# Linear-attention stage on host layouts by token and by dimension: no transposes of k and r, block-diagonal state per head pair, decays on ScalarE

## The reference, cut to what matters

```python
# B=2, H=8, S=768, D=48
for t in range(S):
    kt, vt, rt = k[:, :, t], v[:, :, t], r[:, :, t]
    cur = einsum('bhd,bhe->bhde', u * kt, vt)
    y[:, :, t] = einsum('bhd,bhde->bhe', rt, state + cur)
    state = w * state + einsum('bhd,bhe->bhde', kt, vt)
x = y, as rows of 384 per token          # 1536 tokens
x = moe(x)       # 8 experts of 384x1024 and 1024x384
x = moe2(x)
```

## Time and profile before

| | us |
|---|---|
| median of 3 runs | 395.46 (395.17 to 395.58) |
| the profiled execution's own time | 396.4 |
| its span | 394.3 |
| first score (unit 0) starts at | 15.67 |
| score of unit 2 starts at | 27.98 |
| score of unit 11 starts at | 76.22 |
| one unit from there on, from score to score | 5.36 |
| first expert product starts at | 96.47 |

### The profile page before, as it was taken

The page is one execution under the profiler, slowest core; times in us unless marked ns, Lnnn a source line. Parts: engine busy times, 40 slices in busy tenths (PEclk is TensorE's granted clock), DMA queues, the critical chain, the costliest instruction groups (busy, mean ns, idle before and its releaser), DMA issues.

```text
span 394.3 us, 10784 instructions
## 1 busy us (share of the span) xinstructions
PE 366.7 (93%) x3406; PEld 356.9 (91%) x3407; DVE 209.6 (53%) x539; ACT 133.0 (34%) x230; POOL 184.5 (47%) x303
## 2 busy tenths in 40 slices
PE   4689999988999999999999999879999999999990
PEld 4579999977899999999999999769999999999990
DVE  4356666689688655555555577474214454244210
ACT  2447554410544222222222252105215555255220
POOL 6798999815455532323232334152434524444311
PEclk9999999998999999999999999699999999999996
DMA  6898774146999511111111321139349998492000
GB/s 128 142 353 185 164 161 100 40 129 169 402 405 404 215 40 40 40 40 40 40 40 40 112 114 40 13 82 403 122 153 350 317 327 299 136 345 98 27 23 17
DMA packets 68238, 62.08 MB, mean 157 GB/s; under 512 B 45493, under 2 KB 61028, under 8 KB 68080
## 3 DMA queue, kind: packets, MB, share of 16 engines
q1 hardware_dynamic: 63904, 51.26, 40.9%
q0 software_dynamic: 3744, 10.23, 7.9%
q10 hardware_dynamic: 560, 0.21, 0.2%
HBM read 52.85 MB, written 10.14 MB: 160 GB/s over the span
## 4 chain that ended last, share of the span: by engine, by line
PE 82%; DMA 6%; SPq 4%; DVE 3%; issue 2%; ACT 1%; POOL 1%; ACTq 0%; POOLq 0%; DVEq 0%
PE p_h L1203 35%; PE p_o L1225 28%; DMA w_sb<-in_moe_w 3%; PE p_sc L1118 3%; SPq L406 3%; PE p_x L1090 3%; PE p_xt L1180 2%; PE p_y L1100 2%; PE p_y L1106 2%; DMA w_raw<-in_moe_w 2%; PE p_kv L1081 1%; PE p_kt L1068 1%; PE p_rt L1072 1%; PE p_o L1050 1%; DMA xg<-x_rows,src_idx 1%
## 5 line engine op out<-in xcount | busy, mean ns | idle before, releaser
L1203 PE MATMUL p_h<-xT,w_sb 128*128 128x128 f32 x1296 | 149.3, 275 | 1.6 <-ACT xT L670 1.0
L1203 PEld LDWEIGHTS p_h<-xT,w_sb 128*128 128x128 f32 x1296 | 148.2, 192 | 2.3 <-issue 1.3
L982 DVE SCALAR_TENSOR_TENSOR h_lo<-p_h,h_hi 128x512 fp32r<-128x512 f32 x54 | 37.4, 692 | 78.9 <-ACT h_hi L753 77.8
L999 DVE CUSTOM_DVE_ANT_0 lg_prod<-y_row,wg_all 128x384 f32<-128x384 f32 x112 | 55.8, 554 | 41.9 <-ACT y_row L763 41.7
L1225 PE MATMUL p_o<-w_hi,h_hi 128*128 x216 | 75.4, 349 | 0.0
L1225 PE MATMUL p_o<-w_lo,h_hi 128*128 x216 | 73.1, 339 | 0.0
L1225 PE MATMUL p_o<-w_hi,h_lo 128*128 x216 | 73.0, 338 | 0.0
L753 ACT ACTIVATE h_hi<-p_h 128x512 fp32r<-128x512 f32 x54 | 32.3, 598 | 112.2 <-PE p_h L1203 112.2
L580 POOL TENSOR_TENSOR dst_mark<-zeros 128x1 f32<-128x1 f32 x54 | 15.7, 290 | 105.8 <-DVE y_row L999 68.6
L839 DVE TENSOR_TENSOR w_lo<-w_raw,w_hi 128x1024 fp32r<-128x1024 f32 x36 | 42.0, 1221 | 7.8 <-ACT w_hi L670 7.8
L580 POOL TENSOR_TENSOR src_mark<-zeros 128x1 f32<-128x1 f32 x54 | 18.8, 348 | 49.1 <-PE p_xt L1180 33.9
(11 more groups left out here) (183 smaller groups left out, 408.9 us busy)
## 6 DMA issues: line engine op xcount, KB each, us to landing
w_raw<-in_moe_w SPq DMA_DIRECT2D x12, 1536.0 KB, 9.7
w_sb<-in_moe_w SPq DMA_DIRECT2D x12, 1536.0 KB, 9.5
k_raw<-in_k SPq DMA_DIRECT2D x12, 192.0 KB, 3.2
r_raw<-in_r SPq DMA_DIRECT2D x12, 192.0 KB, 3.6
v_raw<-in_v SPq DMA_DIRECT2D x12, 192.0 KB, 3.8
...
```

The costliest lines, as they stand in the source:

```text
L982: stt(h_lo[:, at, :], p_h[n][:, :, :], 0.0, h_hi[:, at, :].bitcast(F32), ALU.max, ALU.subtract).then_inc(h_ready[layer], 1)
L999: last = nv.tensor_tensor_reduce(out=lg_prod[:, n, :], in0=y_row[par][:, 0:DM], in1=wg2_all[:, e, :], op0=ALU.mult, op1=ALU.add, scale=1.0 ...
L1203: last = mm(p_h[half][:, f, :], w1_sb[place][:, c, col:col + P], xT[:, c, :], start=(c == 0), stop=(c == DC - 1))
```

## The change

The host now hands over other arrays: `rkv` holds r, k and v side by side for each token (1152 numbers), `kr_by_dim` holds k and r with the dimension on the partitions (112 rows of 1024 numbers a unit), `w_by_dim` holds w in 128 rows. SP loads `nat` (128x1152) and `krT` (112x1024) for each unit, two loads in place of three. w_col is loaded without waiting for POOL's clears.

PE's turns of k and r, ACT's three copies of them, r_sc, r_tab and half of the buffers rT go away. DVE scales k and r by dimension in one operation each (kT at L807, rT at L812, 112x512). k by token is scaled too, now on POOL (k_sc, L551), since the product for the state needs it. The state st is block-diagonal for a pair (128x128, zeros outside the blocks), and so the inter part takes 4 matmuls of 128 columns where it took 8 of 64. The decay of the state goes from one DVE operation to eight small ones on ACT (L707, 64x48), and the diagonal is halved between POOL (L544, 128x512) and ACT (L715, four of 128x128). The powers of w grow by doubling (six products). The split of w2 goes behind the attention (`split_high(0, 0)`).

On POOL, the diagonal and the scaling of k:

```diff
-                gp.tensor_tensor(sc[b][:, :, :, :], ident[:, :].unsqueeze(1).unsqueeze(2).broadcast_to([P, 2, HP, T]),
-                                 bonus[:, :].rearrange("p (g j) -> p j g", j=2).unsqueeze(3).broadcast_to([P, 2, HP, T]),
-                                 ALU.mult).then_inc(bonus_diag, 1)
+                gp.tensor_tensor(sc[b][:, 0, :, :], ident[:, :].unsqueeze(1).broadcast_to([P, HP, T]),
+                                 bonus[:, :].rearrange("p (g j) -> p j g", j=2)[:, 0, :].unsqueeze(2).broadcast_to([P, HP, T]),
+                                 ALU.mult).then_inc(diag_pool, 1)
...
+                wait_pos(pool, kv_made, n - 1)
+                gp.tensor_tensor(k_sc[b][:, :, :, 0:D], k_nat(q).rearrange("p (g j) d -> p g j d", j=2),
+                                 k_tab[:, :, :, 0:D], ALU.mult).then_inc(k_scaled, 1)
```

On DVE, the scalings of k and r and the state:

```diff
-                tt(k_sc[b][:, :, :, 0:D], pairs(k_raw[q]), k_tab[:, :, :, 0:D], ALU.mult).then_inc(k_scaled, 1)
+                dve.wait_ge(krT_loaded[q], 16 * (i + 1))
+                wait_pos(dve, scored, n - 1)
+                tt(kT[b][0:R, :, :], krT[q][0:R, 0, :, :], pk[0:R, :, :], ALU.mult).then_inc(kT_ready, 1)
...
+                wait_pos(dve, y_made, n - 1)
+                tt(rT[b][0:R, :, :], krT[q][0:R, 1, :, :], pr[0:R, :, :], ALU.mult).then_inc(rT_ready, 1)
...
-                tt(st_sum[:, :, :], st[b][:, :, 0:D], p_kv, ALU.add).then_inc(state_ready, 1)
+                for j in range(2):
+                    at = rows_of(j)
+                    last = tt(acc[b][at, :, :], st[b][at, :, j, 0:D], p_kv[at, :, :], ALU.add)
+                last.then_inc(summed, 1)
-                tt(st[b][:, :, 0:D], st_sum[:, :, :], decay, ALU.mult).then_inc(state_ready, 1)
```

On ACT, the copies that go, the diagonals and the decays:

```diff
-                copy(kT[0:R, :, :], p_kt[0:R, :, :]).then_inc(kT_ready, 1)
-                for j in range(2):
-                    at = slice(HD * j, HD * j + D)
-                    last = copy(rT[b][at, j, :, :], p_rt[at, :, :])
+                for g in range(HP):
+                    last = sa.activation(sc[b][:, 1, g, :], ident[:, :], ACT.Copy, scale=bonus[:, 2 * g + 1:2 * g + 2])
+                last.then_inc(diag_act, 1)
...
+                act.wait_ge(summed, n + 1)
+                act.wait_ge(y_made, n + 1)
+                for g in range(HP):
+                    for j in range(2):
+                        at = rows_of(j)
+                        last = sa.activation(st[b][at, g, j, 0:D], acc[b][at, g, :], ACT.Copy, scale=w_T[at, g:g + 1])
+                last.then_inc(decayed, 1)
-                if isinstance(n, int) and 0 < n <= NPC:
-                    split_high(0, 0, [n - 1])
```

On PE, the inter part:

```diff
-                    for j in range(2):
-                        mm(p_y[rows_of(j), g, :], st[b][0:R, g, :], rT[b][0:R, j, g, :],
-                           start=(g == 0), stop=False, skip_group_check=True)
+                    mm(p_y[:, g, :], st[b][0:R, g, :, :], rT[b][0:R, g, :],
+                       start=(g == 0), stop=False, skip_group_check=True)
```

More of the change, by code:

```diff
@@ L423, in expert_w2 @@
                     .then_inc(w2_loaded[place], 16)
-            sp.wait_ge(ones_set, 1)
-            sp.wait_ge(zeros_set, 1)
-            with nc.allow_non_contiguous_dma(reason="a few hundred decays, one to a partition"):
-                for j in range(2):
-                    sp.dma_start(w_col[HD * j:HD * j + D, :], w_jd[j]).then_inc(w_loaded, 16)
+            sp.dma_start(w_col[:, :], w_rows).then_inc(w_loaded, 16)
             for q in range(RING):
@@ new lines, in unit @@
+            def unit(i, q, n, b, c):
+                products(i, q, n)
+                if isinstance(n, int) and n == 0:
+                    pool.wait_ge(cleared, 2)
+                    pool.wait_ge(k_tab_ready, 1)
+                    scale_k(q, n, b)
+                else:
+                    diagonal(n, b)
+                    scale_k(q, n, b)
+            pool.wait_ge(u_loaded, 16)
+            units(pool, unit)
+            gp.memset(ones_e[:, :], 1.0)
+            gp.memset(zeros[:, :], 0.0).then_inc(zeros_set, 1)
@@ L572, in _ @@
[L572 to L574 removed]
+            pool.wait_ge(consts, 3)
+            pool.wait_ge(zeros_set, 1)
             def mark(of, signal):
```

331 lines of the change are left out of this document (166 added, 165 removed).

## The result

The change makes the kernel 0.9% slower, which is clear of the noise. The median is 399.41 us (397.07 to 401.89, 11 runs) against 395.64 us (394.59 to 397.02, 11 runs) of the kernel before on the same chip: ratio 1.0086, 95% interval 1.0059 to 1.0114. The prediction was 393.0 with a range up to 397.5, so it named the wrong side, and the time lies outside its range. The profiled execution took 401.89 us, the slowest of the eleven, with a span of 400.2; it lies 5.5 us above the profiled one of before, where the medians are 3.8 apart, so places read from this pair show some 1.7 us more loss than the medians do.

A forecast was written before the change was run, and what follows sets the result against it. PE bounds the kernel before, POOL 0.08 us behind; afterwards POOL's turn, held by DVE, sets 5.5 us a unit. Terms: -7.0 at first score, +4.0 until score 2, +0.5 in the loop: 2.5 faster, 393.0 us; range 388.5 to 397.5.

The forecast's parts named there:

- krT lands at about 6: Start: unit 0's load by dimension lands at about 6 us, at 402 GB/s, giving the first score at 8.7.
- The step from score 0 to score 1, 6.3 us: Start: PE's powers, ACT's copy and diagonals, mask, values and state product lead from score 0 at 8.7 to score 1 at 15.0.
- The clock's price: Rival, between scores 1 and 2: PE's clock halves for 2 to 3 us, 1 to 2 us dearer, 394 to 395; chance 0.13.
- Unit 4's loads: Attention loop: loads average 1.05 MB a unit, 190 GB/s, well under 402, and come four units ahead; no delay counted.
- It was 27.98, late itself, because ACT waited.: Kernel before, score 2: late because ACT waited 3.77 us for w2 ahead of its split; forecast now 25.0, 3.0 us gained.
- the hold: Loop: DVE's SBUF products and POOL's operations wait for each other; POOL's two products held 0.43 and 0.3 us a unit.
- the loop at 5.5: Attention loop: POOL's closed turn through the bonus sum takes 5.5 us a unit, where it was 5.36.
- the half diagonal: POOL in the loop: 512 elements take 1.01 us, half-size by the whole diagonal's rate; at the products' rate 1.28.
- no hold: Rival: DVE and POOL do not hold each other; POOL's turn is 4.8 us and the time 385.3; chance 0.12.
- a decay: ACT in the loop: each of the eight state decays of 48 elements takes 0.21 us.
- ACT becomes the loop: Rival: decays over 0.33 us, diagonals 0.37, make ACT's unit 5.5 or more; 400 us at 0.43 a decay; chance 0.10.
- PE's unit: PE in the loop: 4.44 us a unit without the turns, reached only if nobody else is later.

The follow-up runs named there:

- j2: Changed kernel with unit 0's krT load moved to ACT's DMA queue, behind the bonus table's broadcast load: 401.21 us, ratio 1.0122.
- g2: Changed kernel with unit 0's krT load issued first on ACT's DMA queue, ahead of the bonus table's broadcast: 395.29 us, ratio 0.9981.
- j1: Changed kernel with the bonus table's broadcast load moved to SP's queue, behind both loads of unit 0: 396.73 us, ratio 1.0041.
- h1: Changed kernel with e2's extra warming matmuls and the first expert's loads issued behind the last units' loads: 396.14 us, ratio 1.001.
- h2: Changed kernel with g2's early krT load and the first expert's loads behind the last units' loads: 394.75 us, ratio 0.9999.
- i1: h3 with the changed kernel's own 50 warming matmuls ahead of unit 0 in place of 125: 395.78 us, ratio 1.0009.
- after: The changed kernel itself, against the kernel before: 399.41 us, ratio 1.0086.
- e2: Changed kernel with more warming matmuls (results unread) in PE's early gaps, 125 for 50 ahead of the first score: 399.2 us, ratio 1.0054.
- b1: Kernel before with only the split of the first expert's w2 moved behind the attention: 394.57 us, ratio 0.9963.
- e3: Changed kernel with the two tables of powers that DVE reads placed in PSUM instead of SBUF: 392.51 us, ratio 0.9914.
- h3: Changed kernel with g2's early krT load, late first-expert loads and extra warming matmuls, 125 ahead of unit 0: 398.17 us, ratio 1.0065.
- g3: Changed kernel with PSUM tables, late expert loads, unit 1's bonus sum earlier, warming matmuls and g2's early krT: 385.87 us, ratio 0.9735.

## Why the prediction was wrong, step by step

**The step that failed first: krT lands at about 6.** It took the 402 GB/s of the earlier trace rows for the start and divided the bytes by it. The start moved 101, 138 and 244 GB/s in the three microseconds from 2 to 5, with the table's broadcast in front; j2 and g2, which differ only in whether the table or krT comes first on ACT's queue, have score 0 at 13.81 and 8.11. The prediction listed the bytes of the two loads and left the third out. With krT ahead of the broadcast (g2) scores 0, 1 and 2 come at 8.11, 15.77 and 26.02, where the forecast had 8.7, 15.0 and 25.0. So this step is worth 4.1 of the 5.1 us at score 2. The rate was too high as well: with the broadcast behind both loads (j1) krT still landed at 7.5.

**The step from score 0 to score 1, 6.3 us.** The sum led it through PE's turn and ACT's copy and diagonals alone. At full clock and with a late score 0 that holds, 6.54 in h1. With an early one the other path ends last, 7.66 to 8.58 in g2, h2 and i1: POOL's products wait for the same broadcast load, and DVE's kT stands ahead of the mask, held to 1.48 us in h2 and i1. The sum had neither. That g2's score 2 is within 1.0 us of the forecast is in part luck, since its score 0 came 0.6 us sooner than forecast.

**The clock's price.** The rival was the right mechanism with chance 0.13, at 1 to 2 us, for a half clock of 2 to 3 us. It lasted from some 24.3 to 38 and, around score 0, from some 10.6 to 17.5. The price was 2.1 us from score 2 to 5 and 1.3 from score 0 to 1 (7.84 us in after, 6.54 in e2 and h1 at full clock). In the bubble between scores 1 and 2, where the rival had it, it cost nothing: 10.24 us at either clock. The error was to take the length from the one place in the earlier trace rows, where it was some 3 us, and not to see that a load that lands late makes a second gap ahead of score 0.

**Unit 4's loads.** "DMA has 1.05 MB a unit ... comes four units ahead" was an average; the 3 MB of the first expert stand in the same queue just ahead of unit 4's reload. In after it is hidden behind the clock; it shows in the step from score 3 to 4, 7.22 us in e2 and 8.37 in g2, for 5.5, and in g2 in the next one too, 7.73. No step of the sum had it.

**"It was 27.98, late itself, because ACT waited."** This was right: b1 takes the wait away, and the step from score 1 to 2 falls by 1.85 us.

**Right in mechanism and size:** the hold (e3 shows it); the loop at 5.5 (5.48 to 5.58 measured); kT 1.38 and rT 1.49 for 1.2 and 1.4 with their waits; the half diagonal 1.04 for 1.01; four diagonals on ACT in 1.28 for 1.2; the last unit 4.68 for 4.7; score 2 to 11 in h2 48.71 for 48.7; the split behind the attention hidden (plan_ends 9.87 us behind score 11, as before's 9.85). The rival "no hold" is ruled out.

**Right in kind, off in size:** a decay is 331 ns, not 0.21 us, and eight take 2.75 us. This is the value from which the rival "ACT becomes the loop" was to decide; ACT was busy for 4.87 of 5.48 us, so it did not, but in e3 it is 0.11 us from the end. PE's unit is 4.63, not 4.44: in the chain of after the score takes 1.16 for 1.09 and the rows 1.08 for 0.89, while the inter part takes 0.90 for the 0.98 assumed. It has no effect under 5.5, and is the bound at 4.7 in e3.

**What stays open.** With the load and unit 4 mended (h2) the kernel is level with before, at 394.75, not at 393.0. Score 2 is 1.6 us behind the forecast there and score 11 as much, and the clock explains little of it (i1, at full clock there, has the same delay within 0.3 us): the step from score 0 to 1 is 2.3 us too long and that from 1 to 2 is 0.2, while score 0 is 0.9 early. No edit of after with the loop as forecast had the early load and full clock up to score 11: h3's score 0 was late, and i1's clock fell at 24. g3 had both, with the faster loop. Whether the forecast's time can be met with the loop of 5.5 was not shown. Nor is the spread of after explained (397.07 to 401.89, 1.2%). The clock may have its part in it: it differs between executions with the same work (before and b1 up to score 1, above), and each kernel has only one profiled execution, so a place that one profile gives for a fall is not shown to hold in all.
